# Attention, a routed expert layer and a dense layer in one kernel: six experts taken by falling token count, and their weight splits moved from the attention steps to fixed pairs of the expert stage

## The chip, the cores and the metric

One Trainium2 chip, one of its cores. The metric is the time of one execution on the device in microseconds (us). The kernel before took 907.97 us, the median of three runs (905.46 to 910.26).

## What is computed

Three layers follow each other.

```python
# 1. gated linear attention: 4 x 8 sequences of 768 steps, head size 40
C = f_stab * C + i_stab * outer(v_t, k_t); n = f_stab * n + i_stab * k_t
y_t = sigmoid(o_t) * (C @ q_t) / max(|n . q_t|, 1)
# 2. one expert of eight for each of 3072 tokens (x is 3072 x 320)
e = argmax(x @ w_gate); out = gate_w * (relu(x @ w1[e]) @ w2[e])      # w1[e] 320 x 1024
# 3. dense, 2048 wide
h = x @ w_in; out = max(0.01 * h, h) @ w_out
```

Inputs and outputs are f32. The big products are made in f16 with both operands split into a high and a low part (three products of the four).

## The kernel before, in words

**Weight units.** There are ten: eight experts, and the dense layer cut into two halves of expert size. Splitting a unit takes: a load of its f32 weights into one half of `stage` (A is w1, 320 x 1024; B is w2, 1024 x 320), five squares on ScalarE with an accumulated sum (`square`, L610: three parts of A, two of B), a small matmul that adds the sums over the partitions (`sums`, L1323), a chain of short VectorE operations that makes a power of two of them (`scale`, L834), five high halves on ScalarE (`high`, L622) and five low halves on VectorE (`low`, L875, recorded at L891). The result goes to one of the slots (`slotA`, `slotB`) and from there, for most units, to d_wA and d_wB in device memory.

**Attention, 24 steps** (`step` in every engine's block; six chunks of 128 positions by four batches). A step has three head groups. For each, TensorE makes exponents and scores, ScalarE the exponential, VectorE weighs the scores (`weigh`), TensorE multiplies them with the values, VectorE combines and advances the state. GpSimd gates keys and rows, the x rows go to d_x, and TensorE makes the router logits of the step before last. The weight work is woven in with a cycle of three steps a unit (UP = 3, `job` L641 on ScalarE, `lows` L942 on VectorE, `reload` L394 on the DMA queue of SyncE): squares at the end of the first and the start of the second step, sums and scale at the end of the second (L1323, L834), then the highs, the first two ahead of the next step's first exponential, and the lows, three in the third step and two in the next. Seven units go through it whole (experts 4 to 7, 0, 1 and 2 in this order), the eighth only with its squares. Slots 2 and 3 hold step buffers during attention, so the seventh unit goes into the memory of xreg (slot 4).

**Routing.** VectorE finds for every token its expert, its position among the tokens sorted by expert, and tables for 31 pairs of a tile of 128 sorted tokens and an expert (24 tiles, seven of them at most shared more than once): tab_tile, tab_exp, tab_last (L997 to L1068). It is one chain, each operation waiting for the one before (`rl`). Meanwhile ScalarE makes the highs of the eighth unit and clears Y, which lies in xreg (L702). GpSimd then gathers the rows of a pair from d_x with an indirect DMA (`fetch`, L566).

**Pairs, 31.** For pair p, TensorE runs `h_product` (64 matmuls of 128 columns, L1390, slotA of the expert's parity), then `x_turn` of the next pair (L1380), then `y_product` of the pair before (24 matmuls of 320 columns, L1424, slotB). ScalarE follows with two relus (`h_high`, L715) and the high part of x (`x_high`, L709); VectorE with `h_low` (L1129), `x_low` (L1124), `x_scale` of the pair after next (L1115 to L1119), `y_gate` (L1134) and `y_add` (L1144, whose tile number is loaded from memory at L1140), then its share of weight work. On TensorE the pairs stand in a loop of two (`pairs`, L1461), once for pairs 1 to 10 and once for 11 to 28; between the two come the token table and the sums of the dense units. The other engines have all pairs written out. Both dense units are split here (`dense`, L717 and L1085): squares in pairs 4 to 8, scale in 11, highs in 12 to 16, lows in 13 to 22. SyncE (L443 to L458) stores the eighth unit, loads the dense units, waits for all stores and reloads expert e into slot e % 2 as soon as expert e - 2 is done.

**Dense.** Six groups of four tiles, from slots 2 and 3 (`group`, L1519), written out through GpSimd.

Of the kernel before, what the change touches and what calls it, by code (L numbers as in the profile page):

```python
# [31 lines left out]
ds = bass.ds  # L32
# [32 lines left out]
def build(nc, qkT, k_in, v_in, o_in, ig, fg, wg_in, wA, wB, out):  # L65
    ctx = ExitStack()
    with ctx:
# [13 lines left out]
        d_wA = dram("d_wA", (NE - 2, P, 5 * FE), F16)  # L81
        d_wB = dram("d_wB", (NE - 2, P, NF * 2 * DM), F16)
# [10 lines left out]
        slotA.append(xreg[:, 0:5 * FE // 2].bitcast(F16))  # L93
        slotB.append(xreg[:, 5 * FE // 2:5 * FE // 2 + NF * DM].bitcast(F16))
# [13 lines left out]
        xT = sb("xT", [P, 3, P], F32)  # L108
        wgt = sb("wgt", [P, 3, PVN], F32)
# [4 lines left out]
        zero = sb("zero", [P, 1], F32)  # L114
# [71 lines left out]
        storedA = [sem(f"storedA{i}") for i in range(4)]  # L186
        storedB = [sem(f"storedB{i}") for i in range(4)]
# [5 lines left out]
        rt_tab, rt_a, rt_id, rt_idx = sem("rt_tab"), sem("rt_a"), sem("rt_id"), sem("rt_idx")  # L193
# [28 lines left out]
        qe = q1[:, GH * P:GH * P + NPAIR * NE].rearrange("p (q e) -> p q e", q=NPAIR)  # L222
        plo = sb("plo", [P, NST], F32)
# [7 lines left out]
        lastf = sb("lastf", [P, NE], F32)  # L231
        tab_tile = sb("tab_tile", [P, NPAIR], I32)
# [45 lines left out]
        CONSTS = 19  # L278
# [15 lines left out]

        @block.sync
        def _(sp):
# [7 lines left out]
            def load_A(u):  # L304

                h = u % 2
                a = wA[ds(row(u), 1)].rearrange("a k f -> (a k) f")
                sp.dma_start(stA[h][:, 0:2 * FE].rearrange("p (k f) -> p k f", k=2),
                             a[0:2 * P, :].rearrange("(k p) f -> p k f", p=P)).then_inc(stgA_landed[h], 16)
                for r in range(2):  # L310
                    sp.dma_start(stA[h][r * KR:(r + 1) * KR, 2 * FE:3 * FE], a[2 * P:DM, :]).then_inc(stgA_landed[h], 16)

            def load_B(u):

                h = u % 2
                sp.dma_start(stB[h].rearrange("p (n d) -> p n d", n=NF),
                             wB[ds(row(u), 1)].rearrange("a (n p) d -> p (a n) d", p=P)).then_inc(stgB_landed[h], 16)

            def store_A(u, t):

                sp.wait_ge(lo_done, NSL * u + 3)
                sp.dma_start(d_wA[row(u)], slotA[t][:, :]).then_inc(storedA[2 if t == 4 else t], 16)

            def store_B(u, t):

                sp.wait_ge(lo_done, NSL * (u + 1))
                sp.dma_start(d_wB[row(u)], slotB[t][:, :]).then_inc(storedB[2 if t == 4 else t], 16)
# [52 lines left out]
            load_A(0)  # L380
            load_B(0)
# [12 lines left out]
            def reload(c, b, st):  # L394
# [17 lines left out]
                u = st // UP - 1  # L412
                if st % UP == 1 and 0 <= u < NE - 2:
                    sp.wait_ge(lo_done, NSL * (u + 1))
                    load_A(u + 2)
                if st % UP == 2 and 0 <= u < NE - 2:
                    load_B(u + 2)
                if st % UP == 2 and 0 <= u < NE // 2:
                    store_A(u, slot(u))
                if st % UP == 0 and 0 < u <= NE // 2:  # L420
                    store_B(u - 1, slot(u - 1))
                if st == NST - 2:
                    store_A(NE - 2, slot(NE - 2))
                if st == NST - 1:
                    store_B(NE - 2, slot(NE - 2))
# [9 lines left out]
            load_A(1)  # L435
            load_B(1)
# [4 lines left out]


            store_A(NE - 1, slot(NE - 1))  # L443
            store_B(NE - 1, slot(NE - 1))
            sp.wait_ge(xs_done, 2)
            for u in range(NE, NU):
                load_A(u)
                load_B(u)
            for i in range(4):
                sp.wait_ge(storedA[i], 16 * (2 if i < 2 else 1))  # L450
                sp.wait_ge(storedB[i], 16 * (2 if i < 2 else 1))
# [10 lines left out]
        def _(pool):  # L462
# [20 lines left out]
            const(g.memset(zero[:, :], 0.0))  # L483
# [19 lines left out]
            const(g.iota(rev[:, :], pattern=[[-1, NE]], base=NE, channel_multiplier=0,  # L503
                         allow_small_or_imprecise_dtypes=True))
# [33 lines left out]

            pool.wait_ge(wgc_done, 1)
# [36 lines left out]
            pool.wait_ge(lo_done, NSL * (NE - 2))  # L576
# [20 lines left out]
        def _(act):  # L597
# [12 lines left out]
            def square(u, k):  # L610

                s = u % 2
                x = part(s, k)
                if k == 0:
                    act.wait_ge(stgA_landed[s], 48 * (u // 2 + 1))
                if k == 3:
                    act.wait_ge(stgB_landed[s], 16 * (u // 2 + 1))
                if NSL * u + k >= 2:
                    act.wait_ge(sq_done, NSL * u + k - 1)
                a.activation(dump[(s + k) % 2][:, 0:x.shape[1]], x, ACT.Square, accum_out=sq[:, s, k:k + 1]).then_inc(sq_done, 1)  # L620
# [20 lines left out]
            def job(st, at):  # L641
# [8 lines left out]
                if u >= NE - 1:  # L650
                    return
# [976 lines left out]
```

## Time and profile before

| | |
|---|---|
| profiled execution | 906.79 us, span of its trace 905.0 us |
| three timed runs | 910.26, 907.97, 905.46 us |
| mean granted TensorE clock | 0.965 |
| TensorE matmuls busy | 763.7 us (84%), 6405 |
| VectorE busy | 569.4 us (63%), 1536 |
| ScalarE busy | 361.5 us (40%), 647 |
| GpSimd busy | 157.0 us (17%), 192 |
| DMA | 99.55 MB, mean 110 GB/s |

Busy time is an average over stages which differ: the setup lasts to about 24 us, attention to 272, routing to 301, the pairs to 544 and the dense stage to 905. A wait is ended by the instruction named behind the arrow. A matmul's listed duration holds its way through the array, so consecutive ones overlap.

### The profile page before, as it was taken

The numbers are of one execution on the slowest core, as the hardware profiler recorded it, in microseconds if no ns is written. First come the engines' busy times: TensorE is split into PE (matmuls) and PEld (weight loads), VectorE is DVE, ScalarE is ACT, GpSimd is POOL, SyncE is SP. The second block draws the span as 40 slices with busy tenths as digits, with TensorE's granted clock in tenths as the row PEclk, the third lists the DMA queues.
The fourth block names the chain that finished last, engine by engine and source line by source line (L and its number), as shares of the span: only waits on it lengthen the run. The fifth ranks groups of instructions, "written<-read, shape, count | busy, mean of one in ns | idle before, by whom it ended". The sixth has DMA issues, their size and how long they took to land.

```text
span 905.0 us, 17468 instructions
## 1 busy us (share of the span) xinstructions
PE 763.7 (84%) x6405; PEld 554.4 (61%) x6406; DVE 569.4 (63%) x1536; ACT 361.5 (40%) x647; POOL 157.0 (17%) x192
## 2 busy tenths in 40 slices
PE   0776877776781799999999989999999999999994
PEld 0665765665671687888888875555555555555552
DVE  7677787779788765657776564545545455454341
ACT  2355655655445125325322223343343433433432
POOL 4133343334331111111111000010010010100101
PEclk9999989999895799999999999999999999999997
DMA  4899999996820259333313000000000000000000
GB/s 113 214 255 293 258 323 322 264 307 214 245 97 14 88 178 355 107 114 138 137 31 130 15 3 0 1 15 15 1 30 1 0 29 0 29 0 0 30 1 29
DMA packets 49772, 99.55 MB, mean 110 GB/s; under 512 B 7694, under 2 KB 38094, under 8 KB 46638
## 3 DMA queue, kind: packets, MB, share of 16 engines
q1 hardware_dynamic: 47070, 89.74, 32.0%
q0 software_dynamic: 2640, 9.01, 3.0%
q8 instruction: 34, 0.56, 0.2%
q14 instruction: 28, 0.23, 0.1%
HBM read 74.85 MB, written 23.89 MB: 109 GB/s over the span
## 4 chain that ended last, share of the span: by engine, by line
PE 63%; DVE 17%; issue 10%; ACT 5%; DMA 3%; SPq 1%; POOL 0%; DVEq 0%; ACTq 0%
PE bank L1390 25%; PE bank L1514 13%; PE bank L1424 10%; PE bank L1298 4%; PE bank L1273 3%; DMA slotA<-d_wA 2%; ACT stage L757 2%; DVE qk L1212 2%; DVE slotA L891 1%; PE bank L1282 1%; DVE sxt L1187 1%; ACT stage L774 1%; PE bank L1311 1%; PE bank L1380 1%; PE bank L1290 1%
## 5 line engine op out<-in xcount | busy, mean ns | idle before, releaser
L1390 PE MATMUL bank<-stage,slotA 128*128 128x512 f16 x768 | 181.3, 379 | 0.0
L1514 PE MATMUL bank<-slotB,dec 128*128 128x320 f16 x768 | 159.4, 299 | 15.6 <-DVE qk L1212 13.0
L1207 DVE TENSOR_TENSOR stage<-bank,stage 128x512 f32<-128x512 f32 x96 | 66.3, 691 | 105.4 <-ACT stage L757 105.3
L1390 PE MATMUL bank<-qbd,slotA 128*128 128x128 f16 x1984 | 117.8, 221 | 6.0 <-DVE qbd L1124 3.5
L1390 PEld LDWEIGHTS bank<-qbd,slotA 128*128 128x128 f16 x1984 | 114.9, 99 | 9.4 <-issue 5.4
L1390 PEld LDWEIGHTS bank<-stage,slotA 128*128 128x128 f16 x768 | 75.1, 98 | 74.1
L1514 PE MATMUL bank<-slotB,qk 128*128 128x320 f16 x384 | 114.8, 299 | 0.0
L1514 PEld LDWEIGHTS bank<-slotB,dec 128*128 128x128 f16 x768 | 73.0, 98 | 66.7 <-DVE qk L1212 23.6
L757 ACT ACTIVATE stage<-bank 128x512 f32<-128x512 f32 x96 | 57.4, 598 | 129.1 <-PE bank L1390 129.1
L1424 PE MATMUL bank<-slotB,emov 128*128 128x320 f16 x496 | 102.1, 300 | 4.7 <-issue 3.0
L715 ACT ACTIVATE emov<-bank 128x512 f16<-128x512 f32 x62 | 37.0, 597 | 160.3 <-PE bank L1390 160.3
L1212 DVE TENSOR_TENSOR qk<-stage,dec 128x512 f16<-128x512 f32 x96 | 66.3, 690 | 51.9 <-ACT dec L761 51.9
L761 ACT CAST dec<-stage 128x512 f16<-128x512 f32 x96 | 59.3, 617 | 73.2 <-DVE stage L1207 73.2
L589 POOL DMA_INDIRECT out<-stage,tok_i x24 | 23.6, 983 | 366.9 <-ACT stage L774 362.9
L1129 DVE SCALAR_TENSOR_TENSOR esta<-bank,emov 128x512 f16<-128x512 f32 x62 | 42.6, 689 | 52.2 <-ACT emov L715 52.0
L1424 PE MATMUL bank<-slotB,esta 128*128 128x320 f16 x248 | 74.2, 299 | 0.0
L570 POOL DMA_INDIRECT num<-d_x,idq x31 | 30.8, 995 | 203.2 <-DVE sxi L1119 185.0
L1424 PEld LDWEIGHTS bank<-slotB,emov 128*128 128x128 f16 x496 | 46.0, 98 | 27.7 <-issue 11.0
L620 ACT ACTIVATE slotB<-stage 128x1024 bf16<-128x1024 f32 (+1 forms) x50 | 56.6, 1135 | 5.7 <-DMA stage<-wA 5.1
L671 ACT ACTIVATE dec<-bank 128x384 f32<-128x384 f32 (+1 forms) x72 | 32.3, 449 | 59.1 <-PE bank L1265 58.8
L898 DVE TENSOR_TENSOR dec<-bank,dec 128x384 f32<-128x384 f32 (+1 forms) x72 | 36.3, 504 | 26.5 <-ACT dec L671 25.9
L1514 PEld LDWEIGHTS bank<-slotB,qk 128*128 128x128 f16 x384 | 37.6, 98 | 14.6
(231 smaller groups left out, 1217.1 us busy)
## 6 DMA issues: line engine op xcount, KB each, us to landing
stage<-wB SPq DMA_DIRECT2D x10, 1280.0 KB, 8.1
stage<-wA SPq DMA_DIRECT2D x10, 1024.0 KB, 6.5
slotA<-d_wA SPq DMA_DIRECT2D x6, 1280.0 KB, 6.2
slotB<-d_wB SPq DMA_DIRECT2D x6, 1280.0 KB, 5.8
d_wA<-slotA SPq DMA_DIRECT2D x5, 1280.0 KB, 10.1
d_wB<-slotB SPq DMA_DIRECT2D x5, 1280.0 KB, 6.3
stage<-wA SPq DMA_DIRECT2D x20, 256.0 KB, 8.0
qk<-qkT SPq DMA_DIRECT2D x12, 360.0 KB
```

The source lines that it names most:

```text
L620: a.activation(dump[(s + k) % 2][:, 0:x.shape[1]], x, ACT.Square, accum_out=sq[:, s, k:k + 1]).then_inc(sq_done, 1)
L715: a.activation(hh[i][:, q * 512:(q + 1) * 512], bank[2 * i + q][:, :], ACT.Relu).then_inc(m_hh, 1)
L757: a.activation(ft[f % 2], bank[f % 2][:, :], ACT.Copy, scale=0.01).then_inc(f_t, 1)
L761: a.copy(fhi[f % 2], fgl[f % 2]).then_inc(f_hi, 1)
L898: v.tensor_tensor(dec[i][:, 0:w], psS[i][:, 0:w], dec[i][:, 0:w], ALU.mult).then_inc(p_done, 1)
L1129: v.scalar_tensor_tensor(hl[i][:, q * 512:(q + 1) * 512], bank[2 * i + q][:, :], 0.0, hh[i][:, q * 512:(q + 1) * 512], ALU.max, ALU.subtra ...
L1207: v.tensor_tensor(fgl[f % 2], bank[f % 2][:, :], ft[f % 2], ALU.max).then_inc(f_g, 1)
L1212: v.tensor_tensor(flo[f % 2], fgl[f % 2], fhi[f % 2], ALU.subtract).then_inc(f_lo, 1)
L1298: ins = t_.matmul(psO[i][:, j * PVN:(j + 1) * PVN], dec[i][:, j * P:(j + 1) * P], vv[f][:, h * D1:h * D1 + PVN], start=True, stop=True)
L1390: ins = t_.matmul(pf, a[:, col:col + P], x(k), start=(q == 0), stop=(q == len(ops) - 1))
L1424: ins = t_.matmul(bank[4 + i][:, 0:DM], x[i][:, f * P:(f + 1) * P], slotB[s][:, c0:c0 + DM], start=(f == 0 and q == 0), stop=(f == NF - 1 ...
L1514: ins = t_.matmul(bank[4 + q][:, 0:DM], x[f % 2][:, q * P:(q + 1) * P], slotB[2 + f // NF][:, c0:c0 + DM], start=(f == 0 and z == 0), stop ...
```

## The change

Attention splits only four units: the dense halves (now units 8 and 9), then experts 0 and 1, which stay in slots 0 and 1. The dense halves are stored, and come back to slots 2 and 3 by a reload at pair 25. The six other experts get ranks 2 to 7 by falling token count, worked out in routing (`tab_ord`); SyncE and ScalarE read the rank table to load the right rows. Each rank is loaded, squared, scaled, split and stored at fixed pairs, given by tables. From rank 3 on ScalarE issues the stores and the loads (six DMAs). TensorE's pair loop is cut where sums are made. xreg is cleared once by GpSimd before the first step; `winvp` is made with each scale, and `y_gate` reads the pair's expert number from memory to find it. The logits' copy (`top`) moves ahead of the lows of group 2.

```diff
@@ attention: which step does what @@
-                u, r = st // UP, st % UP
-                if r == 0 and at >= 2:
...
-                    square(u, at - 2)
...
+SPLITS = (8, 9, 0, 1, 2, 3, 4, 5, 6, 7)
+SLOT = (0, 1, 2, 3, 2, 3, 2, 3, 0, 1)
+SQUARES = {(0, 2): (8, 0), (0, 3): (8, 1), (0, 4): (8, 2), (1, 0): (8, 3), (1, 1): (8, 4),
+           (3, 2): (9, 0), (3, 3): (9, 1), (3, 4): (9, 2), (4, 0): (9, 3), (4, 1): (9, 4),
+           (12, 0): (0, 0), (12, 2): (0, 1), (12, 4): (0, 2), (13, 0): (0, 3), (13, 1): (0, 4),
+           (16, 3): (1, 0), (17, 0): (1, 1), (17, 2): (1, 2), (17, 4): (1, 3), (18, 0): (1, 4)}
+HIGHS = {(4, 4): (8, 0), (5, 1): (8, 1), (5, 3): (8, 2), (6, 1): (8, 3), (6, 3): (8, 4),
+         (7, 1): (9, 0), (7, 3): (9, 1), (8, 1): (9, 2), (8, 3): (9, 3), (9, 1): (9, 4),
+         (14, 1): (0, 0), (14, 3): (0, 1), (15, 1): (0, 2), (15, 3): (0, 3), (16, 1): (0, 4),
+         (18, 4): (1, 0), (19, 1): (1, 1), (19, 3): (1, 2), (20, 1): (1, 3), (20, 3): (1, 4)}
+LOWS = {(5, 2): (8, 0), (6, 0): (8, 1), (6, 2): (8, 2), (7, 0): (8, 3), (7, 2): (8, 4),
+        (8, 0): (9, 0), (8, 2): (9, 1), (9, 0): (9, 2), (9, 2): (9, 3), (10, 0): (9, 4),
+        (15, 0): (0, 0), (15, 2): (0, 1), (16, 0): (0, 2), (16, 2): (0, 3), (17, 0): (0, 4),
+        (19, 2): (1, 0), (20, 0): (1, 1), (20, 2): (1, 2), (21, 0): (1, 3), (21, 2): (1, 4)}
+SUMS_AT = {4: 8, 13: 0, 18: 1}
@@ routing, VectorE @@
+            rl(v.tensor_reduce(cnt, r1.rearrange("p (e t) -> p e t", e=NE), AX.X, ALU.add))
+            rl(v.scalar_tensor_tensor(ckey, cnt, float(NE), keyc[:, :], ALU.mult, ALU.add))
+            rl(v.tensor_tensor(above, ckey.unsqueeze(1).broadcast_to(ee), ckey.unsqueeze(2).broadcast_to(ee), ALU.is_gt))
+            rl(v.tensor_reduce(rank, above, AX.X, ALU.add))
...
+            v.tensor_scalar(tab_ord[:, 2:NE], ordf[:, 2:NE], -2.0, None, ALU.add).then_inc(rt_ord, 1)
...
+            rl(v.tensor_tensor(r1.rearrange("p (e t) -> p e t", e=NE), oneh[:, :, :],
+                               rank.unsqueeze(2).broadcast_to([P, NE, NST]), ALU.mult))
+            rl(v.tensor_reduce(tke[:, :], r1.rearrange("p (e t) -> p t e", e=NE), AX.X, ALU.add))
...
-            for to, n, at in ((0, 2, NE - 2), (2, NE - 2, 0)):
-                rl(v.tensor_tensor(winvp[:, to:to + n], winv[:, at:at + n, 0], winv[:, at:at + n, 1], ALU.mult))
...
-            rl(v.tensor_reduce(expf[:, :], qe[:, :, :], AX.X, ALU.add))
@@ pairs @@
+PAIR_SQ = {0: ((3, 0), (3, 1)), 1: ((3, 2), (3, 3), (3, 4)), 4: ((4, 0),), 5: ((4, 1), (4, 2), (4, 3), (4, 4)),
+           9: ((5, 0), (5, 1), (5, 2)), 10: ((5, 3), (5, 4)), 13: ((6, 0), (6, 1), (6, 2)), 14: ((6, 3), (6, 4)),
+           17: ((7, 0), (7, 1), (7, 2)), 18: ((7, 3), (7, 4))}
+PAIR_SCALE = {3: 3, 7: 4, 11: 5, 15: 6, 19: 7}
+PAIR_HI = {3: ((3, 0), (3, 1)), 4: ((3, 2), (3, 3), (3, 4)), 7: ((4, 0), (4, 1), (4, 2)), 8: ((4, 3), (4, 4)),
+           11: ((5, 0), (5, 1), (5, 2)), 12: ((5, 3), (5, 4)), 15: ((6, 0), (6, 1), (6, 2)), 16: ((6, 3), (6, 4)),
+           19: ((7, 0), (7, 1), (7, 2)), 20: ((7, 3), (7, 4))}
+PAIR_LO = {0: ((2, 0), (2, 1)), 1: ((2, 2), (2, 3), (2, 4)), 4: ((3, 0), (3, 1)), 5: ((3, 2), (3, 3), (3, 4)),
+           8: ((4, 0), (4, 1)), 9: ((4, 2), (4, 3)), 10: ((4, 4),), 12: ((5, 0), (5, 1)), 13: ((5, 2), (5, 3)), 14: ((5, 4),),
+           16: ((6, 0), (6, 1)), 17: ((6, 2), (6, 3)), 18: ((6, 4),), 20: ((7, 0), (7, 1)), 21: ((7, 2), (7, 3)), 22: ((7, 4),)}
+PAIR_STORE = {6: 3, 11: 4, 15: 5, 19: 6, 23: 7}
+TOK_AT = 25
@@ ScalarE, after h_high(p) and x_high(p + 1) @@
+            def jobs(p):
+                if p in PAIR_STORE:
+                    x = PAIR_STORE[p]
+                    store_unit(x)
+                    if x + 2 < NE:
+                        load_unit(x + 2)
+                for x, k in PAIR_HI.get(p, ()):
+                    high(x, k)
+                for x, k in PAIR_SQ.get(p, ()):
+                    square(x, k)
+                if p == TOK_AT:
+                    load_dense(0)
+                    load_dense(1)
@@ VectorE, after y_add(p - 1) @@
+            def jobs(p):
+                if p in PAIR_SCALE:
+                    scale(PAIR_SCALE[p])
+                for y, k in PAIR_LO.get(p, ()):
+                    low(y, k)
@@ y_gate @@
-                v.tensor_tensor(gmt[:, p:p + 1], gmt[:, p:p + 1], sxi[:, p:p + 1], ALU.mult)
+                e = dve.value_load(tab_exp[0:1, p:p + 1], min_val=0, max_val=NE - 1)
+                v.scalar_tensor_tensor(gmt[:, p:p + 1], gmt[:, p:p + 1], sxi[:, p:p + 1], winvp[:, ds(e, 1)],
+                                       ALU.mult, ALU.mult)
@@ TensorE @@
-            pairs(1, SCALE_AT)
+            at = 1
+            for p in sorted(PAIR_SCALE):
+                pairs(at, p)
+                sums(PAIR_SCALE[p])
+                at = p
+            pairs(at, TOK_AT)
...
+            pairs(TOK_AT, NPAIR - 2)
@@ GpSimd, before the first step @@
+            g.memset(xreg[:, :], 0.0).then_inc(m_y, 1)
```

Rank 2 is the first: SyncE loads it once `tab_ord` is there, its squares and its sums stand at the end of routing, its scale behind `x_scale(0, 0)`, its highs around the relus of pair 0 and its lows in pairs 0 and 1. `store_unit` waits for the lows of its unit and issues two DMAs, `load_unit` issues four; the first high of a unit waits for its scale. In the diff above, the lines with "@@" only say where it stands.

## Rows read from the trace of the kernel before

**Rows 1.** Windows by stage: length, each engine's busy us, clock, DMA share, GB/s.

```profile
44.20:261.20 217.00, 164.18 (x1257) 138.35 (x1255) 173.34 (x484) 122.58 (x232) 82.84 (x86) 0.95 0.90 269
...
275.00:301.00 26.00, 5.21 (x103) 4.21 (x104) 24.02 (x61) 13.22 (x11) 4.02 (x7) 0.50 0.05 13
308.84:528.70 219.86, 214.08 (x2690) 180.98 (x2691) 139.91 (x431) 67.98 (x117) 26.30 (x27) 1.00 0.38 131
```

**Rows 2.** The same view, single steps: one cycle of three, and step 22.

```profile
199.30:229.80 30.50, 22.23 (x183) 18.61 (x180) 24.64 (x70) 17.54 (x33) 12.35 (x12) 1.00 0.79 229
253.40:261.20 7.80, 7.17 (x65) 6.25 (x63) 6.30 (x23) 5.91 (x15) 3.65 (x5) 1.00 0.46 189
```

**Rows 3.** Timelines of ScalarE and VectorE, 199 to 231: start, length, operation.

```profile
200.69 1.15 ACT L632 ACTIVATE slotA<-stage,wsc 128x1024 f16<-128x1024 f32 x1 [3.53 <-DVE wsc L873]
...
203.71 0.56 DVE L898 TENSOR_TENSOR dec<-bank,dec 128x384 f32<-128x384 f32 x1 [2.99 <-ACT dec L671]
...
206.21 1.91 DVE L891 SCALAR_TENSOR_TENSOR slotA<-stage,wsc,slotA 128x1024 f16<-128x1024 f32 x1
...
216.81 2.17 DVE L891 SCALAR_TENSOR_TENSOR slotB<-stage,wsc,slotB 128x1280 f16<-128x1280 f32 x1
```

**Rows 4.** Chain of waits in the pair stage, and who waited for a reload.

```profile
320.66 3.43 PE bank L1424 x24
324.10 3.57 PE bank L1390 x64
...
336.92 18.41 DMA slotA<-d_wA
...
  PE bank L1390: 1.7, 1
```

**Rows 5.** Timeline of GpSimd in the setup.

```profile
5.94 1.33 POOL L474 MEMSET state<- 128x1476 f32 x1
```

**Rows 6.** Timeline of VectorE in routing.

```profile
275.02 0.36 DVE L998 TENSOR_TENSOR lgs<-lgs,mx 128x192 f32<-128x192 f32 x1
...
280.10 0.62 DVE L1019 TENSOR_REDUCE posf<-qbd 128x24 f32<-128x192 f32 x1
...
281.59 0.17 DVE L1026 TENSOR_SCALAR lastf<-lastf 128x8 f32<-128x8 f32 x1
...
294.25 0.36 DVE L1064 TENSOR_TENSOR winvp<-winv 128x2 f32<-128x2 f32 x2
...
296.35 0.49 DVE L1115 TENSOR_REDUCE sxt<-num 128x1 f32<-128x320 f32 x1
```

**Rows 7.** Landing of the gathers of GpSimd (L570).

```profile
DMA to landing us min/median/max: 2.8/3.0/7.3
```

**Rows 8.** Single lines: squares, highs, lows, min/median/max ns.

```profile
L620 ACT ACTIVATE slotB<-stage x50: 1038/1054/1283, 35.3 to 369.0; 128x1024 bf16<-128x1024 f32 x30, 128x1280 bf16<-128x1280 f32 x20
...
L632 ACT ACTIVATE slotA<-stage,wsc x27: 1131/1138/1162, 45.9 to 423.5; 128x1024 f16<-128x1024 f32 x27
...
L891 DVE SCALAR_TENSOR_TENSOR slotA<-stage,wsc,slotA x27: 1273/1283/1910, 51.4 to 463.8; 128x1024 f16<-128x1024 f32 x18, 64x1024 f16<-64x1024 f32 x9
```

**Rows 9.** Timeline of TensorE where the pair loop is cut.

```profile
386.64 0.37 PE L1476 MATMUL bank<-sq,onesf 128*128 128x10 f32 x2
...
387.92 3.74 PE L1390 MATMUL bank<-qbd,slotA 128*128 128x128 f16 x64 [0.91 <-issue]
```

**Rows 10.** Timeline of VectorE in one pair.

```profile
319.54 0.68 DVE L1129 SCALAR_TENSOR_TENSOR esta<-bank,emov 128x512 f16<-128x512 f32 x1
320.88 0.69 DVE L1129 SCALAR_TENSOR_TENSOR esta<-bank,emov 128x512 f16<-128x512 f32 x1 [0.66 <-ACT emov L715]
...
324.82 0.55 DVE L1144 SCALAR_TENSOR_TENSOR xreg<-bank,gmt,xreg 128x320 f32 x1 [0.85 <-PE bank L1424]
```

**Rows 11.** DMA issues of SyncE: duration of the issuing instruction in ns.

```profile
L456 SPq DMA_DIRECT2D slotA<-d_wA x6: 319/320/5855, 336.9 to 473.3; - x6
...
L311 SPq DMA_DIRECT2D stage<-wA x20: 477/594/1427, 28.0 to 334.4; - x20
```

More of the change, by code:

```diff
@@ L185, in build @@
         hi_done, lo_done = sem("hi_done"), sem("lo_done")
-        storedA = [sem(f"storedA{i}") for i in range(4)]
-        storedB = [sem(f"storedB{i}") for i in range(4)]
+        stored = [sem(f"stored{k}") if k >= 2 else None for k in range(NU)]
+        dense_landed = sem("dense_landed")
         rt = sem("rt")
@@ L222, in build @@
         qe = q1[:, GH * P:GH * P + NPAIR * NE].rearrange("p (q e) -> p q e", q=NPAIR)
+        m0 = GH * P + NPAIR * NE
+        above, shift, isk, tmp8 = (q1[:, m0 + n * NE * NE:m0 + (n + 1) * NE * NE].rearrange("p (e f) -> p e f", e=NE) for n in range(4))
+        m1 = m0 + 4 * NE * NE
+        cnt, ckey, rank, first_at, past, delta, ordf, endk = (q1[:, m1 + n * NE:m1 + (n + 1) * NE] for n in range(8))
         plo = sb("plo", [P, NST], F32)
@@ L440, in _ @@
                 store_x(st, st % NBUF)
[L443 to L451, printed above, removed]
+            sp.wait_ge(rt_ord, 1)
+            for x in range(2, 4):
+                sp.wait_ge(lo_done, lows_until(x - 2))
+                load_A(x)
+                load_B(x)
+            store_A(2)
+            store_B(2)
+            load_A(4)
+            load_B(4)
             sp.wait_ge(rt_tab, 1)
@@ L622, in high @@
-            def high(u, t, k):
-                x = part(u % 2, k)
+                    act.wait_ge(stgB_landed[s], 16 * loads_until(x))
+                n = squares_until(x, k)
+                late = 2 <= x < NE
+                if n >= 2:
+                    act.wait_ge(sq_done, n if late else n - 1)
+                a.activation((late_dump if late else dump[(s + k) % 2])[:, 0:t.shape[1]], t, ACT.Square, accum_out=sq[:, s, k:k + 1]).then_inc(sq_done, 1)
+            def high(x, k):
+                t = part(x % 2, k)
+                n = scale_of(x)
+                if k == 0:
+                    act.wait_ge(sc_chain, scaled(x))
@@ L715, in h_high @@
                     a.activation(hh[i][:, q * 512:(q + 1) * 512], bank[2 * i + q][:, :], ACT.Relu).then_inc(m_hh, 1)
[L717 to L731 removed]
+            def jobs(p):
[5 more added lines that the diff above has]
+                for x, k in PAIR_HI.get(p, ()):
+                    if k == 0 and x >= 4:
+                        act.wait_ge(stored[x - 2], 32)
+                    high(x, k)
+                for x, k in PAIR_SQ.get(p, ()):
[3 more added lines that the diff above has]
+                    load_dense(1)
             x_high(0, 0)
+            for k in range(3):
+                high(2, k)
             h_high(0, 0)
             x_high(1, 1)
+            for k in range(3, NSL):
+                high(2, k)
+            jobs(0)
             for p in range(1, NPAIR - 2):
@@ L738, in _ @@
                 x_high(p + 1, 1 - p % 2)
[L739 removed]
+                jobs(p)
             h_high(NPAIR - 2, 1)
@@ L1145, in y_add @@
                                        ALU.mult, ALU.add).then_inc(m_y, 1)
-            def low3(k):
-                low(NE - 1, slot(NE - 1), k)
             x_scale(0, 0)
-            low3(0)
+            scale(2)
             x_low(0, 0)
@@ L1456, in _ @@
             pe.wait_ge(rt_tab, 1)
+            sums(2)
             x_turn(0, 0)
```

353 lines of the change are left out of this document (171 added, 182 removed).

## The prediction

> **What bounds the kernel now.** I read the windows by stage first [rows 1]. In the twenty-one attention steps 2 to 22 (44.2 to 261.2 us) TensorE is busy 164.2 us of 217.0 and VectorE 173.3; no engine is full. Routing (275 to 301) is nearly all VectorE, 24.0 of 26.0 us. In the pair stage (308.8 to 528.7) TensorE is full, 214.1 of 219.9, while ScalarE is busy 68.0 and VectorE 139.9. The dense stage behind it is not edited. So the change takes work from a stage in which it lies on the path and puts it into one with idle ScalarE time, less idle VectorE time and no idle TensorE time.
>
> Second, the windows of single steps [rows 2]. A cycle of three attention steps carries the split of one unit and takes 30.5 us. The step from 253.4 to 261.2 carries two squares alone and takes 7.8. So a unit costs 30.5 - 3 x 7.8 = 7.1 us. The timeline of VectorE and ScalarE in that cycle says how [rows 3]: ScalarE waits 3.53 us for the scale factors, then does two high halves ahead of the next step's exponentials; VectorE is idle 2.99 us for that, and then low halves of 1.91, 1.28 and 2.17 us stand between the weighings that TensorE waits for. Third, the chain of waits in the pair stage [rows 4]: only TensorE's products, 3.43 us for the second and 3.57 for the first, a pair every 7.5 us, and one exception: the first pair of the third expert waits for its reload, issued at 336.92 and landed 18.4 us later, with TensorE idle for 1.7.
>
> **Attention loses four of its eight splits.** Before, steps 2 to 22 take 217.0 - 21 x 7.8 = 53.2 us over the free step, for seven full splits: 7.6 each. After, four are left: both dense units and experts 0 and 1. Per unit two things differ. The low halves are spread two to a step instead of three and two. They still take 8.2 to 8.8 us of VectorE (three A parts, two B parts, those at group 0 at their longer 1.91 and 2.17 us [rows 3]) over two and a half steps, and a free step leaves VectorE 7.8 - 6.3 = 1.5 us idle [rows 2], so 3.7 us is absorbed: 4.5 to 5.1 left. And only units 8 and 1 wait for a fresh scale, with one high half behind it instead of two, about 2 us each; half a us for the second squares. That makes 19.4 + 4 + 1.5 = 25 us. Saved: 53.2 - 25 = **28 us**. Bounds: at the old 7.6 a unit, 53.2 - 30.4 = 23; with only 4 us a unit, 37. The clearing of xreg moves to GpSimd before step 0, where it waits anyway (it has nothing before the first keys): nothing; uncovered it would be about 7 us, from the 1.33 us clearing of state, 5.2 times as large [rows 5]. Loads and stores fall in number. Nothing for them.
>
> **Routing gets a rank computation.** Before the gather indices VectorE gets one 192-element reduction and one 192-element add (0.36 each [rows 6]), nine operations on 64 elements, four on 8 (0.17), one more 192-element product and one strided reduction like the 0.62 one. A 64-element one lies between 0.18 and 0.36, I take 0.23; each link adds 0.035: 0.8 + 9 x 0.26 + 4 x 0.21 + 0.4 + 0.65 = 5.0 us, all on the chain. Behind the table the two winvp products and the three wide operations go, 294.25 to 296.35: -2.1. The scale of rank 2 (seven short operations, 1.3 us) takes the place of a 1.28 us low half before x_low. ScalarE's last highs and the clearing by ScalarE go, and five squares come, after a load that starts behind the rank; both have over 10 us. Two unit loads (5.2 MB) now run just before the first gather, which lands in 2.8 to 7.3 us [rows 7]; its slack is now near nothing, 0 to 4 us. Routing: **+3 us**, bounds +2 and +7.
>
> **The pair stage gets six splits for two and a bit**: 15 squares, 20 highs and 15 lows more, at 1.05, 1.14 and 1.28 us for an A part and a fifth more for a B part [rows 8]; a square's sum is read out in another 0.19.
> First, TensorE's pair loop is cut at pairs 3, 7, 11, 15, 19 and 25 instead of at 11 alone. The one cut of before shows the price [rows 9]: 0.37 us for the sums and 0.91 idle by "issue" until the product restarts, 1.3 us. Five more cuts, **+6.5**; bounds 3 (cover by waiting) and 8.
> Second, VectorE. A pair takes it, run without a wait, from 319.54 (first h_low) to 325.29 (y_add started plus 0.47) less 0.66 of waiting, some 5.2 us [rows 10]. y_gate gets a load of the expert number from memory. No row shows this load ahead of y_gate; one of its kind stands ahead of y_add at 324.82, with VectorE idle for 0.85 us. Part lies beside x_scale's last operations, which nothing waits on: 0 to 0.85, I take 0.4. A split cycle of four pairs then asks 4 x 5.6 + 6.9 (lows) + 1.3 (scale) = 30.6 of 4 x 7.45 + 1.3 = 31.1 us. It fits on average only, and the waits between the two relu halves (0.66 at 320.88) don't go. Where two or three lows follow each other the next x_low comes late, and the next product with it. A cycle can lose between nothing (backlog worked off in the next pair) and all four waits of 0.66 plus the scale of 1.3, 3.9 us. I take the middle, 2 us, for five cycles: **+10**; bounds 0 and 20.
> Third, ScalarE: 6.6 squares + 6.1 highs + 3 to 5 of DMA issue + 4 x 1.5 of its own (68.0 less 25 for ten squares and ten highs, over 29 pairs) = 22 to 24 of 31 us. In a cut pair the highs wait for the scale, which VectorE makes only after the last y_add (5.6 us past the first product); that is part of the 2 us. Its six DMA issues at pairs 6, 11, 15, 19 hold back the relus behind them. A quiet issue takes 0.32 us (store) to 0.6 (part of a load), 3 in sum [rows 11]. The Trainium skill, "DMA: Bandwidth & Descriptors", section on issuing engines, says that issuing from more engines only saves the sequencer's issue time, "usually small relative to the DMA itself"; by it the term is nothing. The sum, from the quiet issues, takes nothing either; but one issue of before took 5.86 us (a rival below).
> Fourth, the reload of rank 2 is stored by pair 2 and due at pair 7: the 1.7 us wait goes. The others: from the reference's data the experts have 457, 267, 303, 329, 332, 498, 464 and 422 tokens, so ranks 2 to 7 begin at pairs 7, 12, 17, 21, 25 and 28; the last lows of ranks 3 to 7 are at 5, 10, 14, 18, 22, so five pairs (37 us) or more are left for a store and a reload. The dense units' reload at pair 25 has 35 us. The slowest reload of before took 18.4 [rows 4]. Nothing; if a store and a reload both took twice that, 36 us of cover would be gone and the excess would show as a wait of TensorE.
>
> **Sum**: -28 + 3 + 6.5 + 10 - 1.7 = -10.2. The profiled execution took 906.8 us (span 905.0); 896.6, which against the median 908.0 is some 897.
>
> **Rivals.**
> *All is hidden in the pairs.* The backlog is worked off and half the cuts are covered by waits: -28 + 3 + 3 - 1.7 = -23.7, 884 us. For it: VectorE fits on average. Against: 97% full leaves no room. 0.2.
> *Slower: DMA issue blocks ScalarE.* Place: pairs 6, 11, 15, 19, 23. Between two needs ScalarE has the y product (3.43), the next first product (3.57) and y again (3.43), less 1.5 for its own pair work, 0.7 for the VectorE operation behind it and 1.1 until it is free: 7.1 us. In pairs 11, 15 and 19 three highs (3.4) share it, so issues of more than 3.7 us in sum delay the products. If the last of the six waits as the 5.86 us one did and another half as long, the sum is 10 to 11: 3 x 6.5 + 2 x 3.1 = 26 us more, 922 us. For it: that one issue, and 1.43 us for one that is 0.6 otherwise [rows 11]. Against: they were the tenth and the fourth transfer of a queue; here six follow each other. 0.15.
> *Nothing is won in attention.* Its steps are bound by TensorE and its chain, not by the splits: 0 + 3 + 6.5 - 1.7, 915 us. The step of 7.8 us against 10.2 speaks against it. [...] 0.05.
> *Half and half*: attention saves the lower 23 and the backlog is 15: 906.8 - 23 + 3 + 6.5 + 15 - 1.7 = 906.6. 0.1.
>
> **Chances and range.** The forecast, 885 to 905, has 0.5. Half a per cent (4.5 us) is about what a measurement can tell here, so faster means below 903.5: 0.2 and nine tenths of 0.5, 0.65. Slower, above 912.5: the blocked and the attention rival, 0.2. The same: 0.15. The range leaves out the far ends of the bounds and takes in the hidden case and most of the way to the blocked one: 881 to 914; the forecast's own is 885 to 905.
>
> **What would show it.** Right: step windows near 9.6 us where two lows fall and 7.8 in steps 11 and 23, the last step's scores some 28 us earlier than 261.2; gather indices some 5 us later behind the last logits; first products' spacing 7.45 in quiet pairs and 8.5 to 9.5 in one or two pairs of each cycle, ended by x_low; a restart gap near 1 us at six places. Wrong: steps that stay above 10 us; relus waiting on ScalarE's DMA issue; a product waiting for a reload; spacing of 7.45 throughout.

## The result: 0.46% slower, with the gain in attention more than spent in the pairs and the setup

The changed kernel takes 910.7 us (median of 16 runs, 907.4 to 913.6) against 906.4 for the kernel before in the same comparison: ratio 1.0046, 95% interval 1.0032 to 1.0061. The forecast was 897. The profiled execution spans 909.2 us (before: 905.0).

The windows by stage, of the kernel after: steps 2 to 22 of attention, the pairs from product 1 to product 30 (as in [rows 1]), then step 22, step 6 and step 3 (as in [rows 2]).

```profile
52.10:230.10 178.00, 154.50 (x1248) 133.59 (x1246) 147.39 (x444) 85.75 (x176) 72.15 (x84) 0.97 0.75 217
283.17:532.75 249.58, 221.94 (x2697) 186.27 (x2698) 167.73 (x478) 103.57 (x163) 26.30 (x27) 0.98 0.59 213
222.80:230.10 7.30, 7.17 (x63) 6.20 (x61) 6.95 (x23) 2.25 (x6) 2.93 (x4) 1.00 0.07 25
88.20:96.33 8.13, 7.09 (x63) 6.19 (x60) 7.83 (x20) 4.75 (x8) 4.00 (x5) 1.00 0.53 149
58.97:71.02 12.05, 7.31 (x63) 6.36 (x60) 5.93 (x22) 5.36 (x12) 2.14 (x3) 0.88 0.98 245
```

Attention fell from 217.0 to 178.0 us over these steps (37.5 from the first scores to those of step 23), more than forecast. The pairs rose from 219.9 to 249.6. The first scores start at 30.5 us instead of 24.1 (+6.4), and from the scores of step 23 to the first product it takes 44.7 us instead of 39.6 (+5.1). With +0.4 for the first pair and +29.8 from product 1 to product 28 (235.1 instead of 205.3): 6.4 - 37.5 + 5.1 + 0.4 + 29.8 = +4.2, the difference of the spans. Here and below, "product 9" is the first product (`h_product`) of pair 9.

The setup, in the timelines of GpSimd and VectorE of the kernel after (start, length, operation); in the kernel before, the same TENSOR_SCALAR took 0.20 us at 11.41.

```profile
11.55 6.49 POOL L554 MEMSET xreg<- 128x7680 f32 x1
...
11.44 0.15 DVE L842 TENSOR_TENSOR gm<-slotB,slotA 32x1 f32<-32x1 f32 x1
11.62 6.45 DVE L844 TENSOR_SCALAR gnl<-slotB 32x6 f32<-32x6 f32 x1
18.11 0.55 DVE L849 TENSOR_SCALAR slotB<-slotB 32x768 bf16<-32x768 f32 x1
```

A TENSOR_SCALAR on 32x6 elements lasts as long as GpSimd's clear beside it, and ScalarE's exponentials wait for it. The Trainium skill, "SBUF — State Buffer", section "SBUF: two separate sides", describes one port pair shared by GpSimd and by those VectorE operations that use a second port: whichever starts first holds it for its whole instruction. By that rule the small operation stands until the clear ends, and these rows agree (both end at 18.0 to 18.1); they do not show which ports it uses.

Who TensorE waited for in the pairs (products 1 to 28: us in all, times, longest). Before, first fence; after, second.

```profile
PE bank L1424 <- issue: 2.3, 10, 0.3
PE bank L1390 <- DVE qbd L1124: 1.9, 1, 1.9
PE bank L1390 <- DMA slotA<-d_wA: 1.7, 1, 1.7
PE bank L1390 <- issue: 0.9, 1, 0.9
```

```profile
PE bank L1420 <- issue: 9.9, 7, 3.3
PE bank L1420 <- DVE qbd L1156: 9.4, 6, 2.3
PE bank L1454 <- issue: 7.7, 14, 1.4
PE bank L1454 <- DVE xreg L1178: 1.3, 1, 1.3
```

TensorE's waits rise by 22 us. The wait for the reload [rows 4] is gone; waits for x_low (qbd) come, as forecast (7.5 of the 9.4 us, since one of 1.9 was there before), but the larger part is put down to "issue". Beyond the waits, products 4, 9 and 21 take 5.37 us instead of 3.74, each behind an idle of 2.3 to 3.3 us; the window of product 9, in the kernel after, shows a granted clock of 0.67 over its length, part of it at the lower level of 1.2 GHz ("half clock" below).

```profile
354.52:359.67 5.15, 5.15 (x63) 5.15 (x64) 3.66 (x5) 0.60 (x1) 0.89 (x1) 0.67 0.55 185
```

(The window is 0.22 us shorter than the product.) That is 3 x 1.63 = 4.9 us more. One cycle shows the form of the lateness: timelines of ScalarE, VectorE and TensorE of the kernel after, pairs 11 and 12.

```profile
376.89 0.47 ACT L739 CAST qbd<-bank 128x384 f16<-128x384 f32 x1
377.13 1.55 ACTq L727 DMA_DIRECT2D d_wB<-slotB  x1
...
380.55 2.72 ACTq L719 DMA_DIRECT2D stage<-wA  x2
383.37 0.59 ACTq L720 DMA_DIRECT2D stage<-wB  x1
384.60 3.23 ACT L653 ACTIVATE slotA<-stage,wsc 128x1024 f16<-128x1024 f32 x3 [7.23 <-DVE winvp L901]
387.73 1.05 ACT L745 ACTIVATE emov<-bank 128x512 f16<-128x512 f32 x2
...
380.74 0.22 DVE L1167 SCALAR_TENSOR_TENSOR gmt<-gmt,sxi,winvp 128x1 f32<-128x1 f32 x1 [0.70 <-issue]
382.47 0.55 DVE L1178 SCALAR_TENSOR_TENSOR xreg<-bank,gmt,xreg 128x320 f32 x1 [1.51 <-issue]
...
384.05 0.16 DVE L901 TENSOR_TENSOR winvp<-winv 128x1 f32<-128x1 f32 x1
388.42 1.29 DVE L1161 SCALAR_TENSOR_TENSOR esta<-bank,emov 128x512 f16<-128x512 f32 x2 [4.21 <-ACT emov L745]
389.62 0.55 DVE L1156 TENSOR_TENSOR qbd<-bank,qbd 128x384 f16<-128x384 f32 x1
...
380.33 3.74 PE L1420 MATMUL bank<-qbd,slotA 128*128 128x128 f16 x64
385.37 0.44 PE L1454 MATMUL bank<-slotB,emov 128*128 128x320 f16 x2 [0.97 <-issue]
390.78 0.40 PE L1420 MATMUL bank<-qbd,slotA 128*128 128x128 f16 x4 [1.98 <-DVE qbd L1156]
```

Product 12 ends at 383.9. Its relus start at 387.73, because ScalarE first issues six transfers (376.7 to 384.0) and then makes three highs, and the highs wait for the scale chain, which VectorE has put behind y_add. VectorE, named as the releaser of product 13, was idle for 4.21 us itself: it is not backlogged here, it waits in a ring: VectorE's chain, ScalarE's highs and relus, VectorE's x_low, the next product. (Product 7 is otherwise: VectorE works without a break on lows up to 332.4 and on h_low and x_low up to 334.1, and the product starts at 334.56, 1.18 us late. That is the forecast's backlog.) The chain is late for one more reason. y_gate and y_add (L1167, L1178) each load a number from memory first. The idle before them is 0.14 and 0.85 us in quiet pairs, but 0.7 and 1.5 us in pairs 6, 11, 15, 19 and 23, and at least as long there in e2 (below), where ScalarE issues nothing. What makes it longer there stays open.

### The profile page after: what moved, and what is told of

The parts are those of the page before. It is cut to its first block, busy times and chain, and to the rows that moved or that the text cites. A ratio compares the mean times of both kernels' runs of the same rounds, so it can differ in the third digit from the quotient of the medians.

```text
span 909.2 us, 17693 instructions
## 1 busy us (share of the span) xinstructions
PE 763.1 (84%) x6405; PEld 557.0 (61%) x6406; DVE 579.7 (64%) x1554; ACT 358.9 (39%) x643; POOL 154.3 (17%) x195
## 4 chain that ended last, share of the span: by engine, by line
PE 46%; DVE 23%; DMA 10%; issue 9%; ACT 6%; SPq 3%; ACTq 1%; DVEq 1%; POOL 0%; POOLq 0%
PE bank L1420 20%; PE bank L1547 12%; PE bank L1454 5%; DMA d_x<-slotA 3%; DMA stage<-wB 2%; PE bank L1325 2%; ACT stage L793 2%; PE bank L1300 2%; DMA d_x<-og 2%; DVE qk L1240 2%; DVE slotA L920 2%; DVE slotB L920 2%; DVE esta L1161 1%; DVE stage L1235 1%; DVE sxt L1215 1%
## 5 line engine op out<-in xcount | busy, mean ns | idle before, releaser
L1420 PE MATMUL bank<-qbd,slotA 128*128 128x128 f16 x1984 | 123.2, 226 | 20.9 <-DVE qbd L1156 11.0
L1420 PEld LDWEIGHTS bank<-qbd,slotA 128*128 128x128 f16 x1984 | 119.3, 102 | 25.6 <-issue 24.4
L653 ACT ACTIVATE slotA<-stage,wsc 128x1024 f16<-128x1024 f32 x30 | 33.2, 1140 | 40.6 <-DVE winvp L901 40.6
## 6 DMA issues: line engine op xcount, KB each, us to landing
slotB<-d_wB SPq DMA_DIRECT2D x6, 1280.0 KB, 11.8
```

The costliest lines, as they stand in the source:

```text
L653: a.activation(o_, t, ACT.Copy, scale=sc).then_inc(hi_done, 1)
L1420: ins = t_.matmul(pf, a[:, col:col + P], x(k), start=(q == 0), stop=(q == len(ops) - 1))
```

## The experiments

All times stand against the kernel before, run beside each on the same chip (906.4 to 908.1). "Against after" is the difference of two such ratios times 907; its own interval is some 2 to 3 us wide each way. A trace is one execution, so a figure read from one can differ from the median by a few us.

**e1_clear.** The clear moves from GpSimd's setup to ScalarE in routing.

```
-            g.memset(xreg[:, :], 0.0).then_inc(m_y, 1)
...
+            a.copy(xreg[:, :], zero[:, :].broadcast_to([P, NST * DM])).then_inc(m_y, 1)
             act.wait_ge(pv_done, NG * NST)
```

> The changed kernel with one edit: the 128x7680 clear of the accumulators leaves GpSimd's setup and is made by ScalarE after the routing's exponential, where ScalarE waits 13.3 us for the weights of rank 0. Theory of the setup (GpSimd's 6.49 us clear holds VectorE's 32x6 TENSOR_SCALAR for 6.45 us, and with it the chain to step 0): the scores of step 0 start at about 24.1 instead of 30.5 us, the TENSOR_SCALAR takes about 0.2 us, and the kernel is 6.4 us faster than the changed kernel (about 904 us). Rival (as forecast, the clear lies beside other work and the later start has another cause, such as the landing of the gates): no change, 910.7 us. If ScalarE's clear delays the routing, up to 6 us of the gain goes back there.

Measured 905.55, ratio 0.9976 (0.9960 to 0.9992): 6.4 us less than after. In its timelines the operation is short, and the clear takes 6.57 us of an idle ScalarE:

```profile
11.49 0.16 DVE L846 TENSOR_SCALAR gnl<-slotB 32x6 f32<-32x6 f32 x1
...
241.27 6.57 ACT L707 COPY xreg<-zero 128x7680 f32<-128x7680 f32 x1
```

So the setup theory holds, and this edit alone brings the change to 2 us ahead of the kernel before.

**e5_cuts.** The kernel before, with the loop cut as after.

```
-            pairs(1, SCALE_AT)
+            pairs(1, 3)
+            pairs(3, 7)
+            pairs(7, SCALE_AT)
...
-            pairs(SCALE_AT, NPAIR - 2)
+            pairs(SCALE_AT, 15)
+            pairs(15, 19)
+            pairs(19, 25)
+            pairs(25, NPAIR - 2)
```

> The kernel before with nothing but the loop of pairs cut in the same places as in the changed kernel (3, 7, 15, 19 and 25 beside its own cut at 11), with no sums in them. Forecast's price: 5 x 1.3 = 6.5 us or less, as the sums are not there, 910 to 913 us. Theory of the code (2.9 us for each boundary): 14 us, about 920 us. Rival (boundaries cost nothing, the changed kernel's idle time there is VectorE's): within 1 us of 906.4 us.

Measured 913.23, ratio 1.0058 (1.0044 to 1.0072): +5.3 us. That is near the forecast's price in sum, and 2.9 us for a cut is refuted, here. But the time is not lost where the forecast had it, between the end of one loop and the first product of the next. Products 3, 15, 19 and 25, each the first of a new loop, have no idle before them (product 7 waits for a reload in both kernels); the idle stands before product 4 (0.48), 5 (0.95) and 9 (1.77) and in pair 16 (1.1). Products 9 and 15 of e5:

```profile
374.23 3.74 PE L1390 MATMUL bank<-qbd,slotA 128*128 128x128 f16 x64 [1.77 <-issue]
...
421.73 3.74 PE L1390 MATMUL bank<-qbd,slotA 128*128 128x128 f16 x64
```

Products 5, 9 and 17 begin the second round of their loops. What [rows 9] priced (0.37 us for the sums, 0.91 of idle behind them) belongs to a place with sums; e5 has none at its new cuts, and e9 below shows this idle without a new loop. So the agreement of 5.3 with 6.5 is a coincidence of two different costs.

Each new loop is one more copy of the loop's code. The page of the profile counts what is fetched: queue q8 carries 34 packets in the kernel before, and here

```profile
q8 instruction: 49, 0.80, 0.4%
```

as many as after. The Trainium skill, "Runtime: NRT & Kernel Launch", section "Instruction fetch mechanics", says that crossing a block of code is mostly hidden, but that a taken branch to code that is not there stalls. The rows agree with the first half (no idle at the entry of a new loop); that the idle before products 5 and 9, which follow a branch back, is such a stall fits both: one packet of q8 falls into the idle before product 9 (372.4 to 374.3 us), none into 405 to 427 us, where product 15 starts on time. That the packet makes the idle is argued, not shown.

**e3_loop.** The changed kernel with pairs 3 to 22 in one nested loop; `two(p)` is the old loop body.

```
-                pairs(at, p)
-                sums(PAIR_SCALE[p])
...
+            pairs(1, 3)
+            with pe.Fori(0, 5) as r:
+                pe.wait_ge(sq_done, r * 5 + 30)
+                t_.matmul(psT[:, SUMS:SUMS + NSL], onesf[:, :], sq[:, 0, :], start=True, stop=True).then_inc(sqr_done, 1)
+                with pe.Fori(0, 2) as s:
+                    two(r * 4 + s * 2 + 3)
+            pairs(23, TOK_AT)
```

> The changed kernel with TensorE's pairs 3 to 22 in one nested loop that holds the sums of ranks 3 to 7 (five of the sums' matmuls as before, but four loop boundaries fewer and one more, at 23). Theory of the code (each loop boundary makes TensorE fetch its instructions anew, 2.9 us each where the forecast had 1.3): 3 boundaries fewer give 8 to 10 us, about 902 us, fewer instruction-fetch packets (about 34 to 40 instead of 49), and idle before the h products at 7, 11, 15 and 19 of under 0.5 us. Forecast's price of a cut: 3 x 1.3 = 4 us, about 907 us. Rival (VectorE's backlog fills what the boundaries leave): under 2 us, 909 us or more.

Measured 909.58, ratio 1.0019 (1.0008 to 1.0029): 2.4 us less than after, not 8 to 10. The packets fell to 40 as expected, yet 1.2 to 1.3 us of idle stayed before products 11, 15 and 19. No new loop's code begins there in e3; the sums still stand there.

**e2_sync.** The changed kernel with its stores, loads and dense reloads issued by SyncE, each store behind the reload of the rank before. (With very uneven experts this order could wait for itself; these token counts don't.)

```
                 sp.dma_start(slotB[e % 2][:, :], d_wB[e - 2]).then_inc(wB_landed[e % 2], 16)
+                if e + 1 < NE:
+                    sp.wait_ge(lo_done, lows_until(e + 1))
+                    sp.dma_start(d_wA[e - 1], slotA[SLOT[e + 1]][:, :]).then_inc(stored[e + 1], 16)
+                    sp.dma_start(d_wB[e - 1], slotB[SLOT[e + 1]][:, :]).then_inc(stored[e + 1], 16)
+                if e + 3 < NE:
+                    load_A(e + 3)
+                    load_B(e + 3)
```

> The changed kernel with ScalarE's stores and loads of the experts' weights issued by SyncE, between its reloads, with the same waits on the data. Forecast's term (issuing costs ScalarE nothing that the pairs see): within 1 us of the changed kernel, 910.7 us. Rival of the forecast (ScalarE blocked by its issues): 10 us or more faster, 900 us. Theory after the traces (ScalarE held 6.6 us at pair 6 and 3 to 5 us at pairs 11 and 15, hidden in part): 2 to 5 us faster, 906 to 908 us.

Measured 911.35, ratio 1.0042 (1.0026 to 1.0058): no change. Alone, this would confirm the forecast's "nothing" for ScalarE's issues. But in its timeline the highs of pair 11 start at 385.06, against 384.60 after, and wait still for the scale:

```profile
385.06 3.23 ACT L664 ACTIVATE slotA<-stage,wsc 128x1024 f16<-128x1024 f32 x3 [7.79 <-DVE winvp L880]
```

The issues were covered by the late chain. The sum also hides two effects: in the profiles, product 1 to product 25 takes 2.6 us longer than after (product 13 ran at half clock, 5.37 us), and product 26 to 27 takes 7.40 us instead of 8.75, since the reloads of the dense weights at pair 25 are part of this edit.

**e6_scale** and **e7_both.** VectorE takes the scale chain ahead of y_gate and y_add; e7 with e2's edit too.

```
                 x_scale(p + 2, i)
+                if p in PAIR_SCALE:
+                    scale(PAIR_SCALE[p])
                 y_gate(p - 1)
...
-                if p in PAIR_SCALE:
-                    scale(PAIR_SCALE[p])
```

> The changed kernel with one edit: in the pairs VectorE takes the scale chain of a rank ahead of y_gate and y_add of the pair before instead of behind them. Theory (the wait ring: y_add waits for the product before, the scale chain stands behind it, three highs of 3.2 us on ScalarE wait for the chain and stand ahead of the next relu, so h_low and x_low come late and TensorE idles before h9, h13, h17 and h21 and the y products between, 11 us, and two of these h products run at half clock, 3 us): highs start about 2 us earlier at each of the five places; where ScalarE issues no transfers (pairs 3, 7) the idle goes, at 11 and 15 its issues of 6.6 us still hold the highs; together 5 to 9 us faster than the changed kernel, 902 to 906 us. Forecast's account (the idle is VectorE's own backlog of lows): no change, 911 us, as VectorE's work is the same.

> Both edits: the scale chain ahead of y_gate, and the stores and loads of the weights issued by SyncE, which alone changed nothing. Theory (two causes of one lateness on ScalarE, the chain and the issues, each hides the other): more than the sum of the two alone, 10 to 14 us faster than the changed kernel, 898 to 901 us, h9, h13, h17 and h21 with under 0.5 us idle before them, and no h product at half clock but h4. Rival (the issues never matter): the same as with the scale chain alone. Forecast's account: no change, 911 us.

Measured 907.21, ratio 1.0002 (0.9982 to 1.0022), 4.0 us less than after; and 903.93, ratio 0.9956 (0.9937 to 0.9975), 8.2 less. So 0.4 and 4.0 apart, 8.2 together; the intervals are some 2 us wide each way, so that the two interact is likely here and shown below. Worked out from the timelines, the first high starts so many us after the product of its pair:

| pair | after | e2 | e6 | e7 |
|---|---|---|---|---|
| 7 | 12.2 | 11.4 | 10.1 | 9.3 |
| 11 | 12.0 | 12.5 | 11.2 | 8.7 |
| 15 | 11.7 | 12.6 | 12.4 | 8.7 |
| 19 | 11.8 | 11.8 | 8.8 | 8.7 |

At pair 19, where a store alone is issued, the chain's place does all; at 11 and 15 both have to go. (The trace of e6 is of an execution of 911.27 us, 4 us above its median; its product 15 took 5.37 us, which is part of the 12.4.) My expectation for e7 was 3 us or more too good: product 9 still starts 3.33 us late, now with every operand ready.

```profile
354.86 1.39 PE L1399 MATMUL bank<-qbd,slotA 128*128 128x128 f16 x20 [3.33 <-issue]
```

**e8_all** adds e3's loop and e1's clear to e7; **e9_oneloop** puts pairs 1 to 24 into one nested loop.

```
+            with pe.Fori(0, 6) as r:
+                with pe.Fori(0, 2) as s:
+                    with pe.If(s == 1):
+                        with pe.If(r < 5):
...
+                    two(r * 4 + s * 2 + 1)
```

> Both edits with the nested loop for pairs 3 to 22 and the clear of the accumulators on ScalarE. If the effects add (clear 6.3 us, nested loop 2.5 us as measured alone): about 9 us below the kernel with both edits, 889 to 892 us, which would beat the kernel before by 15 us or more. If the nested loop's gain was only a filling of idle time that the scale chain made, 1 to 2 us more than that.

> As the one before, with pairs 1 to 24 in one nested loop in which the sums stand under two conditions, so that the cuts at 3 and at 23 go too. Theory (the 2.4 us of idle before h4 and its half clock, and the 0.6 us before h3, come from code of a second loop that TensorE has not fetched yet): 3 to 5 us faster than the one before, 886 to 888 us. Rival (the idle before h4 waits for data, or the conditions cost what the cuts did): within 1.5 us of it.

Measured 890.48, ratio 0.9811 (0.9790 to 0.9832), and 885.76, ratio 0.9762 (0.9741 to 0.9783). From e7 to e8 13.1 us go, of which the clear has 6.4: the loop that was worth 2.4 alone is worth 6.8 once ScalarE is in time. Product 9 of e8, and the page of e9:

```profile
345.81 3.74 PE L1402 MATMUL bank<-qbd,slotA 128*128 128x128 f16 x64
```

```profile
q8 instruction: 34, 0.56, 0.3%
```

Product 9 has no wait at all, so its 3.3 us in e7 came with the loop that is entered at 7, whose second round it begins; e5, which has the same loop without this chain, shows 1.77 there. (The traces give 5.0 us for products 1 to 28 from e7 to e8, less than the 6.8 of the medians.) e9 takes 4.4 us more off: in after, e3, e6 and e8 product 4 waited 2.4 to 2.7 us and then ran at half clock, 1.5 to 1.6 us longer. (The cut at 3 is not the whole cause, as e5 has it and waits 0.48 us there.) In e9 no product from 1 to 28 is longer than 3.75 us, and q8 carries no packet from 300 to 470 us (pairs 4 to 24), while in e7 one lies between 349 and 351.5 us, where the idle before product 9 begins.

One idle is left in e9, at the places of the sums, though no loop begins there. Pair 15:

```profile
389.82 0.39 PE L1489 MATMUL bank<-sq,onesf 128*128 128x5 f32 x2
391.40 3.74 PE L1402 MATMUL bank<-qbd,slotA 128*128 128x128 f16 x64 [1.20 <-issue]
```

It is 1.00 at 11 and 1.05 at 19. From the product before the sums to the one behind them it takes 8.8 to 9.0 us at these three places, 1.4 to 1.6 more than the 7.45 of a quiet pair; for the five new places that makes an estimate of some 7 us. Whether the sums or the branches beside them make the idle was not tried.

**e13_act_issue.** e9 with ScalarE's issues back.

> The kernel with one loop, the scale chain first and the clear on ScalarE (885.8 us with SyncE's issue), with the stores and loads issued by ScalarE again. Theory (ScalarE's 6.6 us of issue stand ahead of three highs at pairs 11 and 15, and nothing else hides them now): h13 and h17 get 1 to 2 us of idle each and the pairs before them come late, 3 to 6 us slower, 889 to 892 us. Forecast's account (issuing costs ScalarE nothing that the pairs see): 886 us.

Measured 892.60, ratio 0.9827 (0.9802 to 0.9853): 5.9 us slower than e9 (3 us wide each way), as the theory said. The edit that moved nothing in e2 is worth about six here, but only part of it is the ring. In the profiles, product 1 to 28 takes 7.1 us longer: 3.5 up to product 25, and 3.6 from product 26 to 27, where the dense weights come back. In the ring the mechanism is to be seen: the first highs of pairs 11 and 15 start 11.2 and 10.8 us after their product instead of 8.7, and products 13 and 17 come 1.5 and 1.3 us later. So an interaction is shown (up to product 25 the same edit costs 2.6 us in e2 and gives 3.5 here), but the price of ScalarE's issues in the ring is some 3.5 us and not 5.9.

**e11_spread.** e9 with a low half of pairs 1 and 5 put one pair later, and two squares of pair 5.

```
-PAIR_LO = {0: ((2, 0), (2, 1)), 1: ((2, 2), (2, 3), (2, 4)), 4: ((3, 0), (3, 1)), 5: ((3, 2), (3, 3), (3, 4)),
+PAIR_LO = {0: ((2, 0), (2, 1)), 1: ((2, 2), (2, 3)), 2: ((2, 4),), 4: ((3, 0), (3, 1)), 5: ((3, 2), (3, 3)), 6: ((3, 4),),
```

> The fastest kernel so far (one loop, SyncE's issue, scale chain first, clear on ScalarE) with the third low half of pairs 1 and 5 put into pairs 2 and 6 and two squares of rank 4 put into pair 6. Theory (VectorE's three lows at pair 5 make x_low late for the product of pair 7, 1.4 us, and the y product of pair 6, 1.2 us; those of pair 1 the 0.8 us before h3): 2 to 3 us faster, 883 us. Rival (the idle there is from the relu behind ScalarE's squares or from the load of the expert number): within 1 us, 886 us.

Measured 885.21, ratio 0.9764 (0.9743 to 0.9784): not to be told from e9. Products 1 to 28 took 1.2 us less in the profiles, too little for the theory.

**e10_top_late** and **e12_top_early.** The changed kernel also copies the router's logits (`top`) ahead of the low half at group 2, which the forecast did not price. e10 puts it back to the step's end; e12 does it early in the kernel before.

```
-                    if g == 2 and st >= 2:
-                        top(st - 2)
                     lows(st, g)
+                if st >= 2:
+                    top(st - 2)
```

> The changed kernel with the copy of the router's logits (top) put back where the kernel before has it, at the end of VectorE's step behind the low halves, instead of ahead of them. Theory (TensorE's transposes of the step after wait for this copy, so its place and not the number of splits is what shortened the free steps from 7.8 to 6.9 or 7.3 us): the free steps 2, 11, 12 and 22 go back to about 7.8 us, those with a low at group 2 lengthen by up to 1.3 us, and the kernel is 10 to 18 us slower than the changed one, 920 to 928 us. Rival (the place of the copy does not matter, the steps are shorter because the splits are gone): within 2 us, 909 to 913 us.

> The kernel before with nothing but that copy put ahead of the low halves at group 2, as the changed kernel has it. Theory of its place: 8 to 15 us faster than the kernel before (892 to 899 us), steps 10 and 22 near 7.0 us instead of 7.8. Rival: within 2 us of it, 905 to 909 us, steps as before.

Measured 918.02, ratio 1.0120 (1.0095 to 1.0146), 6.7 us more than after; and 907.18, ratio 0.9999 (0.9985 to 1.0014), nothing. Both are less than expected. Of the free steps 2, 11 and 12 did not change (step 12 takes 6.8 us in e10, too), while step 22, behind a step with a low half at group 2, takes 8.6 instead of 7.3. Step 6, with a low half at group 2, takes 8.90 instead of 8.13.

```profile
87.40:96.30 8.90, 7.34 (x64) 6.25 (x61) 8.01 (x21) 4.76 (x8) 4.11 (x5) 1.00 0.54 147
142.10:148.90 6.80, 6.80 (x62) 6.06 (x60) 5.36 (x20) 4.81 (x11) 2.73 (x4) 1.00 0.96 318
```

So the early copy is worth 6.7 us with the new spread of lows and nothing with the old one. Steps with two lows take 8.8 to 9.9 us in e10, around the 9.6 that the forecast gave for them, and 7.7 to 9.0 after. Why free steps take 6.9 to 7.3 us and not 7.8 stays open; it is not the squares that the step of 7.8 carried, as step 12 carries three.

## Why the forecast was wrong, step by step

**Attention, -28:** right in mechanism, too small: 37.5, just past the bound of 37. The early copy has 6.7 of the 9.5 missed. Free steps shorter than the 7.8 us of [rows 2] have the rest; steps 3 and 13, at 12.1 and 10.2 us, went the other way: they waited 4.7 and 3.0 us for a load of v.

**The clear on GpSimd, "nothing":** wrong by 6.4. The text named the uncovered price, about 7 us, but looked only at what GpSimd waited for and not at which engine shares its time.

**Routing, +3:** 5.1, within its bounds.

**The cuts, +6.5:** the number met a cost that it did not describe, and left one out. The 1.3 us a place were read at a place with sums and belong to such places: they are still there in e9, some 7 us by the estimate above, where no loop is cut but at 25. The cuts themselves, without sums, cost another 5.3 us (e5), later in the loops, above all at the product that begins a second round: 1.8 us at product 9 there, 3.3 in e7. That term stood at nothing.

**VectorE's backlog, +10, and ScalarE's issues, 0:** the main step that failed. The size of the x_low waits is near (7.5 us more than before), but the backlog is the reason at products 3 and 7 alone (1.9 us); 5.6 us at 13, 17 and 21 are the ring. The forecast counted VectorE's time (30.6 of 31.1 us a cycle) and took the scale behind y_add as "part of the 2 us", and the issues as nothing. The chain's place and ScalarE's issues hold three highs back, so that the relus of pair 12 start 7.4 us behind the start of their product instead of 4.3 (e9); each covered the other, and both covered part of the cuts. Their edits with the loops are worth 8.2 + 6.8 + 4.4 = 19.4 us together, where each alone gives 0.4, 4.0 and 2.4 (the single loop was not tried alone). Part of the 8.2 is no ring but the other issuer of the dense reloads (about 1 us from product 26 to 27, e6 against e7). The rival "DMA issue blocks ScalarE" had the right places in pairs 11 and 15, at a fraction of its price (5.9 us in all and 3.5 in the ring, for 26). The quiet issues gave 3 us [rows 11]; with the loads of row numbers between them they took 6.6 at pair 6 and 7.2 at pair 11. The Trainium skill, "DMA: Bandwidth & Descriptors", section "Issuing engines are not separate DMA queues", calls the issue "usually small relative to the DMA itself". That is so here too (the last of the six, issued at 383.37, landed 20.2 us later), but it says nothing of what stands behind the issue on its engine, and the forecast's "nothing" did not follow from it. y_gate's load, put at 0.4 us, takes 0.14 in quiet pairs.

**The reload wait, -1.7:** right.

The forecast's sum of -10.2 becomes +4.2 with +6.4 for the clear, +15.0 for the pairs (29.8 instead of 14.8), +2.5 for routing and the first pair, and -9.5 for attention. It is luck that the error is 14 us and not 24, since the gain missed in attention offsets 9.5. (Its 896.6, put against the median of 908.0, is 897.8 and not 897.)

## What to carry to other kernels

When a side engine gets new work, follow the ring through it and not its busy share: which wait does the new work stand behind, and what stands behind the new work? A chain on which another engine waits goes ahead of the operation that waits for TensorE; that was one moved line. An edit undone alone gives only what nothing else covers: undo the suspects together before one is cleared. A price read at one place holds for all that stands there: ask which part of it the change repeats. And when a test meets the forecast's number, look in its trace whether the time is lost at the forecast's place. With its four faults mended (the clear, the chain's place, the issues, the loops) the changed kernel beats both, 885.8 us against 907.

## What the hardware showed that was not expected

A GpSimd clear of 6.49 us held a VectorE operation of 0.2 us for 6.45. A new loop did not delay its first product (e5: no idle before products 3, 15, 19 and 25), but in e5 five of them cost 5.3 us in all, with 0.95 and 1.77 us of idle before the products that begin a second round at 5 and 9; in e7 the idle at second rounds is 1.1 to 3.3 us at 5, 9, 13 and 17. The instruction queue carried 49, 40 and 34 packets for seven, four and two loops. In e13 the dense reloads at pair 25 kept the transfers near 400 GB/s, and from product 26 to product 27 it took 11.1 us instead of 7.5 (e9), with gaps by "issue" inside TensorE's transposes; whether its code fetch queued behind these transfers was not tried.
